# Issuing first-layer and second-layer matmuls alternately in a fused attention and expert-network kernel

## The chip, the cores and the metric

The kernel runs on one core of one Trainium2 chip. It is a single launch that computes everything. The metric is device time in microseconds; three runs of the kernel before gave 687.64, 683.81 and 687.77 us, median 687.64.

## What is computed

The reference has three parts, chained. Retention-like attention over 2 batches, 8 heads, 576 positions, head size 64 gives x, 1152 tokens by 512 features. Then four experts and one more network, each of two layers, run over all tokens:

```python
scores = scale * np.matmul(q, k.transpose(0, 1, 3, 2))
out    = np.matmul(scores * Dmat[None], v)          # Dmat: causal decay
# x is (1152, 512); four experts, w1 (512, 1024), w2 (1024, 512)
h = np.maximum(x @ w1[e], 0.0)
out += p[:, e:e + 1] * (h @ w2[e])
# then one network, w_in (512, 2048), w_out (2048, 512)
h = x @ w_in
sp = np.where(h > 20.0, h, np.log1p(np.exp(np.minimum(h, 20.0))))
g = h * np.tanh(sp)
out = g @ w_out
```

All inputs and outputs are float32.

## The kernel before, in words

**Tiling.** After attention the kernel treats the rest as six experts (EXPERTS): 0 to 3 are the four experts, 4 and 5 the two halves of the last network. Each has 1024 hidden features, cut into 8 units of 128 (UNITS). The 1152 tokens are cut into three chunks of 384 (PH, TC). A *tile* is one unit for one chunk: 24 tiles in an expert (TPE), numbered n = 8 c + t for chunk c and unit t.

**Two layers of a tile.** The first layer (`hidden`) multiplies the weights of the unit with the 512 features of x in four pieces and accumulates 128 hidden features by 384 tokens in one of four banks of PSUM, banks 4 to 7 (`ps_h`), by turns. The second layer (`project`) multiplies the 128 hidden features with the second weights and adds to four output pieces in banks 0 to 3 (`ps_acc`), which collect all eight units of a chunk. Every operand is held as a sum of two parts, `_hi` (rounded) and `_lo` (the rest), so each product is three matmuls of 128x128 by 128x384 (`three`, L265 to L267): hi by hi, hi by lo, lo by hi. A layer of a tile is 4 x 3 = 12 matmuls, all alike in size.

**Between the layers, experts 0 to 3.** VectorE computes relu times the expert's probability out of PSUM (h_act, L531), ScalarE rounds it to h_hi (L416), VectorE subtracts for h_lo (L525). VectorE does this tile by tile (`moe_tile`). After the tile numbered 8 (c+1) + 2, it adds the four accumulators of chunk c to acc_sb (`add_up`, L546, L548).

**Between the layers, experts 4 and 5.** The activation takes more steps: ScalarE m_u (L438), VectorE m_a and m_w (L596, L598), ScalarE m_r twice (L443, L445), GpSimd m_t (L686), VectorE m_c, m_n, h_act (L605, L611, L614), then h_hi and h_lo. The engines are two tiles ahead in a software pipeline. VectorE's order for tile n is

```python
mish_c(n, e)
mish_out(n, e)          # m_n, h_act
mish_w(n + 2, e)        # m_a, m_w of a later tile
lo(n, e)                # h_lo
```

and ScalarE's is m_u of n+2, h_hi of n, m_r of n+2. In the first tile of a chunk `add_up` of the chunk before follows `lo`. GpSimd also makes the low part of each weight unit (w_lo, L191), ScalarE the high part (w_hi, L186), eight of each per expert.

**TensorE's order.** TensorE is three tiles ahead with the first layer (AHEAD): in the loop over experts, chunks and units it issues `hidden` of tile n+3 and then `project` of tile n. I call this pair a *block*. `hidden` waits until its PSUM bank was read (s_hf), and for weights (s_wl) and x (s_ph) where these are new; `project` waits for h_lo (s_hl), and in the first tile of a chunk, before each output piece, until its accumulator was read (s_af). At the end of `hidden` s_g1 is raised, for ScalarE or VectorE; at the end of `project` s_g2. Each engine runs its instructions in the order in which they are written.

Of the kernel before, what the change touches and what calls it, by code (L numbers as in the profile page):

```python
# [29 lines left out]
P = 128  # L30
# [13 lines left out]
UNITS = 8  # L44
EXPERTS = MOE_EXPERTS + MLP_F // (UNITS * P)
TC = 384
PH = TOKENS // TC
TPE = PH * UNITS
KT = DM // P
UW = KT * P + DM  # L50
RAW = 4
HR = 4
# [9 lines left out]
def build(nc, qk_in, kv_in, row_decay_in, key_decay_in, mask_in, probs_in, weights_in, probs_dram, out_t):  # L62
    with ExitStack() as ctx:
        def sb(name, shape, dt=F32, stack=ctx):
            return stack.enter_context(nc.sbuf_tensor(name, shape, dt))

        def sem(name):
            return ctx.enter_context(nc.semaphore(name))
# [5 lines left out]
        x_hi = sb("x_hi", [P, KT, TOKENS], F32R)  # L74
        x_lo = sb("x_lo", [P, KT, TOKENS], F32R)
# [28 lines left out]
        h_hi = sb("h_hi", [P, HR, TC], F32R)  # L104
        h_lo = sb("h_lo", [P, HR, TC], F32R)
# [16 lines left out]
        ps_acc = [banks[d][:, 0:TC] for d in range(KT)]  # L122
        ps_h = [banks[4 + i][:, 0:TC] for i in range(HR)]
# [27 lines left out]
        s_g1 = sem("s_g1")  # L151
        s_acc = sem("s_acc")
        s_g2 = sem("s_g2")
        s_hf = sem("s_hf")
        s_hh = sem("s_hh")
        s_hl = sem("s_hl")
        s_af = sem("s_af")
# [12 lines left out]
        def cols(c):  # L170
            return slice(c * TC, (c + 1) * TC)

        def high(u):
            return w_hi0[:, u] if u < RAW else w_hi1[:, u - RAW]

        def low(u):
            return w_lo0[:, u] if u < RAW else w_lo1[:, u - RAW]
# [72 lines left out]
        @block.tensor  # L250
        def _(pe):
            def scores(b, n):

                slot, par = n % SLOTS, n % 2
                pe.wait_ge(s_qd, 2 * CHUNKS * b + 2 * (n + 1))
                for y in range(2):
                    for i in range(HALF):
                        hp = HALF * y + i
                        mm = pe.matmul(ps_s[par][y][:, i], qk[:, slot, 1, hp, :], q_diag[:, par, hp],  # L259
                                       start=True, stop=True)  # L260
                    mm.then_inc(s_sc, 1)

            def three(out, w, x, first, last):

                pe.matmul(out, w[0], x[0], start=first, stop=False)  # L265
                pe.matmul(out, w[0], x[1], start=False, stop=False)  # L266
                return pe.matmul(out, w[1], x[0], start=False, stop=last)  # L267

            def unit(u, at):

                return high(u)[:, at:at + P], low(u)[:, at:at + P]

            def hidden_products(c, t):

                for k in range(KT):
                    mm = three(ps_h[t % HR], unit(t, P * k), (x_hi[:, k, cols(c)], x_lo[:, k, cols(c)]),
                               k == 0, k == KT - 1)
                mm.then_inc(s_g1, 1)


            pe.wait_ge(s_zt, 1)
            for _ in range(WARM):
                pe.matmul(banks[7][:, :], zeros[:, 0:P], zeros[:, :], start=True, stop=True)
            scores(0, 0)
            with pe.Fori(0, BATCH) as b:
                for c in range(CHUNKS):
                    slot, par = c % SLOTS, c % 2
                    pe.wait_ge(s_vd, CHUNKS * b + c + 1)
                    if c > 0:

                        pe.wait_ge(s_st, 2 * (CHUNKS - 1) * b + 2 * c)
                    if c + 1 < CHUNKS:
                        for hp in range(PAIRS):
                            for x in range(2):
                                head = slice(DH * (2 * hp + x), DH * (2 * hp + x + 1))
                                mm = pe.matmul(ps_state[DH * x:DH * (x + 1), hp, :], kv[:, slot, 0, head],
                                               kv[:, slot, 1, head],
                                               start=(c == 0 and hp == 0), stop=True, skip_group_check=True)
                        mm.then_inc(s_kvp, 1)
                        scores(b, c + 1)  # L300
                    else:
                        with pe.If(b < BATCH - 1):
                            scores(b, c + 1)
                        with pe.If(b == BATCH - 1):


                            pe.wait_ge(s_xl, TC // CH)
                            pe.wait_ge(s_wl, AHEAD)
                            for t in range(AHEAD - 1):
                                hidden_products(0, t)  # L310
                    for y in range(2):
                        pe.wait_ge(s_sm, 2 * CHUNKS * b + 2 * c + y + 1)
                        for hp in range(HALF * y, HALF * (y + 1)):
                            for x in range(2):
                                h = 2 * hp + x
                                mm = pe.matmul(ps_o[par][DH * x:DH * (x + 1), hp, :],  # L316
                                               kv[:, slot, 1, DH * h:DH * (h + 1)],
                                               s_masked[:, par, hp, x, :],
                                               start=(hp == 0), stop=True, skip_group_check=True)
                    if c > 0:  # L320
                        for hp in range(PAIRS):
                            mm = pe.matmul(ps_o[par][:, hp, :], state[:, 1 - par, hp, :], qk[:, slot, 0, hp, :],  # L322
                                           start=False, stop=True, skip_group_check=True)
                    mm.then_inc(s_o, 1)
            pe.drain().then_inc(s_g2, UNITS)
            pe.wait_ge(s_xt, STEPS - 1)
            hidden_products(0, AHEAD - 1)

            def hidden(e, c, t):

                if t == 0:
                    pe.wait_ge(s_ph, PH * e + (c + 1))
                if c == 0:
                    pe.wait_ge(s_wl, UNITS * e + (t + 1))
                pe.wait_ge(s_hf, TPE * e + (UNITS * c + t + 1))
                hidden_products(c, t)

            def project(e, c, t):

                pe.wait_ge(s_hl, TPE * e + (UNITS * c + t + 1))  # L340
                for d in range(KT):
                    if t == 0:
                        pe.wait_ge(s_af, PH * KT * e + (KT * c + d + 1))
                    mm = three(ps_acc[d], unit(t, KT * P + P * d), (h_hi[:, t % HR, :], h_lo[:, t % HR, :]),
                               t == 0, t == UNITS - 1)
                    if t == UNITS - 1 and d < KT - 1:
                        mm.then_inc(s_acc, 1)
                mm.then_inc(s_g2, 1)

            with pe.Fori(0, EXPERTS) as e:  # L350
                for c in range(PH):
                    for t in range(UNITS):
                        n = UNITS * c + t + AHEAD

                        if n < TPE - 1:
                            hidden(e, n // UNITS, n % UNITS)
                        if n == TPE - 2:
                            hidden(e, PH - 1, UNITS - 1)
                        if n >= TPE:
                            with pe.If(e < EXPERTS - 1):  # L360
                                hidden(e + 1, 0, n - TPE)
                        project(e, c, t)


        @block.scalar
# [387 lines left out]
```

## Time and profile before

| | |
|---|---|
| three runs, median | 687.64 us (683.81 to 687.77) |
| profiled execution: span, first to last instruction | 682.0 us (no other time is given for it) |
| attention, loading, first tiles | until about 66 us |
| experts 0 to 3 | about 66 to 467 us |
| experts 4 and 5 | about 467 to 682 us |
| TensorE busy | 657.8 us, 96% |
| VectorE busy | 362.5 us, 53% |
| granted clock of TensorE, mean | 0.997 |

The profile names matmuls by line and operands: `x_hi,w_hi`, `x_lo,w_hi`, `x_hi,w_lo` are first layer, `h_hi,w_hi`, `h_lo,w_hi`, `h_hi,w_lo` second layer; the bank's number is left out. A matmul's length is modelled (0.33 to 0.34 us), and the next one starts before its end, so the distance from start to start, the pitch, is what counts. "Idle before, releaser" in square brackets is how long the engine stood and whose instruction ended it. PEld is the weight load that goes with each matmul.

### The profile page before, as it was taken

What the parts mean: (1) busy time and instruction counts of PE and PEld (TensorE: products, weight loads), DVE (VectorE), ACT (ScalarE), POOL (GpSimd) and SP (SyncE); (2) the same over time, 40 slices, a digit from 0 to 9 for tenths busy, and PEclk for the clock granted to TensorE, in tenths of its full rate; (3) what the DMA queues carried; (4) which work ended last, traced back from release to release, by engine and by line L of the source; (5) the groups of instructions that cost most, each with busy time, mean ns of one, the idle gap of its engine ahead of it and who ended that gap; (6) DMA issues with size and microseconds to landing.
All of it is one profiled execution on the core that took longest, in us unless ns stands there. A gap on an engine that the chain in (4) does not pass through costs nothing.

```text
span 682.0 us, 10838 instructions
## 1 busy us (share of the span) xinstructions
PE 657.8 (96%) x3993; PEld 643.8 (94%) x3993; DVE 362.5 (53%) x618; ACT 225.8 (33%) x405; POOL 187.2 (27%) x113
## 2 busy tenths in 40 slices
PE   8979999999999999999999999999899998799998
PEld 5868999999999999999999999999899997699997
DVE  5534532325232334232344242547997789988786
ACT  4554211133111133111133121235555454444442
POOL 2255400046000056000055000153423256532222
PEclk9989999999999999999999999999999999999999
DMA  9994300023000023000024000031100002001011
GB/s 276 293 281 167 123 1 1 1 93 124 31 0 0 0 92 134 20 0 0 0 93 153 0 0 0 0 122 63 62 0 0 0 31 92 0 0 46 0 46 46
DMA packets 13967, 40.78 MB, mean 60 GB/s; under 512 B 2304, under 2 KB 4608, under 8 KB 13952
## 3 DMA queue, kind: packets, MB, share of 16 engines
q1 hardware_dynamic: 12848, 38.22, 17.5%
q10 hardware_dynamic: 1104, 2.38, 1.1%
q8 instruction: 7, 0.11, 0.1%
q14 instruction: 8, 0.07, 0.0%
HBM read 38.22 MB, written 2.38 MB: 60 GB/s over the span
## 4 chain that ended last, share of the span: by engine, by line
PE 84%; DVE 7%; DMA 4%; ACT 2%; issue 2%; SPq 1%; DVEq 0%; ACTq 0%
PE bank L265 27%; PE bank L267 27%; PE bank L266 27%; DMA qk<-in_qk 4%; DVE m_a L596 3%; PE bank L259 1%; PE bank L322 1%; DVE m_c L605 1%; PE bank L316 1%; DVE m_w L598 1%; ACT m_u L438 1%; ACT w_hi L186 1%; DVE acc_sb L548 1%; ACT m_r L443 1%; DVE h_lo L525 1%
## 5 line engine op out<-in xcount | busy, mean ns | idle before, releaser
L265 PE MATMUL bank<-h_hi,w_hi 128*128 128x384 f32 x576 | 195.4, 339 | 12.9 <-DVE h_lo L525 11.3
L191 POOL TENSOR_TENSOR w_lo<-w_raw,w_hi 128x1024 fp32r<-128x1024 f32 x48 | 117.9, 2461 | 323.0 <-ACT w_hi L186 322.8
L266 PE MATMUL bank<-h_lo,w_hi 128*128 128x384 f32 x576 | 194.0, 337 | 0.0
L267 PE MATMUL bank<-h_hi,w_lo 128*128 128x384 f32 x576 | 194.0, 337 | 0.0
L267 PE MATMUL bank<-x_hi,w_lo 128*128 128x384 f32 x576 | 194.0, 337 | 0.0
L265 PE MATMUL bank<-x_hi,w_hi 128*128 128x384 f32 x576 | 193.7, 336 | 0.1
L266 PE MATMUL bank<-x_lo,w_hi 128*128 128x384 f32 x576 | 193.5, 336 | 0.0
L416 ACT ACTIVATE h_hi<-h_act 128x384 fp32r<-128x384 f32 x144 | 75.2, 522 | 290.2 <-DVE h_act L531 269.0
L531 DVE SCALAR_TENSOR_TENSOR h_act<-bank,pb 128x384 f32<-128x384 f32 x96 | 53.5, 557 | 178.8 <-PE bank L267 178.2
L525 DVE TENSOR_TENSOR h_lo<-h_act,h_hi 128x384 fp32r<-128x384 f32 x144 | 97.4, 676 | 67.2 <-ACT h_hi L416 67.2
L265 PEld LDWEIGHTS bank<-h_hi,w_hi 128*128 128x128 f32 x576 | 108.0, 187 | 16.9 <-DVE h_lo L525 13.8
L265 PEld LDWEIGHTS bank<-x_hi,w_hi 128*128 128x128 f32 x576 | 108.1, 188 | 0.3 <-issue 0.3
L266 PEld LDWEIGHTS bank<-x_lo,w_hi 128*128 128x128 f32 x576 | 108.2, 188 | 0.0
L266 PEld LDWEIGHTS bank<-h_lo,w_hi 128*128 128x128 f32 x576 | 108.1, 188 | 0.0
L267 PEld LDWEIGHTS bank<-x_hi,w_lo 128*128 128x128 f32 x576 | 108.1, 188 | 0.0
L267 PEld LDWEIGHTS bank<-h_hi,w_lo 128*128 128x128 f32 x576 | 108.0, 188 | 0.0
L686 POOL TENSOR_TENSOR m_t<-m_w,m_r 128x384 f32<-128x384 f32 x48 | 56.2, 1171 | 130.1 <-ACT m_r L445 130.1
L186 ACT ACTIVATE w_hi<-w_raw 128x1024 fp32r<-128x1024 f32 x48 | 50.7, 1056 | 34.3 <-PE bank L267 34.2
L596 DVE TENSOR_SCALAR m_a<-m_u 128x384 f32<-128x384 f32 x48 | 37.2, 775 | 29.8 <-ACT m_u L438 29.8
L443 ACT ACTIVATE m_r<-m_w 128x384 f32<-128x384 f32 x48 | 25.2, 526 | 46.6 <-DVE m_w L598 46.6
L438 ACT ACTIVATE m_u<-bank 128x384 f32<-128x384 f32 x48 | 23.3, 485 | 43.6 <-PE bank L267 43.6
L605 DVE SCALAR_TENSOR_TENSOR m_c<-m_r,m_t 128x384 f32<-128x384 f32 x48 | 30.7, 640 | 1.1 <-POOL m_t L686 0.3
(37 smaller groups left out, 321.3 us busy)
## 6 DMA issues: line engine op xcount, KB each, us to landing
w_raw<-in_weights SPq DMA_DIRECT2D x48, 512.0 KB, 3.3
qk<-in_qk SPq DMA_DIRECT2D x12, 384.0 KB, 13.3
kv<-in_kv SPq DMA_DIRECT2D x12, 384.0 KB, 14.6
pb<-probs_by_expert ACTq DMA_DIRECT2D x4, 576.0 KB, 8.9
out_t<-acc_sb SPq DMA_DIRECT2D x2, 768.0 KB, 3.6
row_decay<-in_row_decay SPq DMA_DIRECT2D x6, 192.0 KB, 7.6
out_t<-acc_sb SPq DMA_DIRECT2D x4, 192.0 KB, 1.9
mask<-in_mask SPq DMA_DIRECT2D x1, 36.0 KB, 3.7
```

Source lines behind the costliest of these rows:

```text
L186: act.activation(high(u), w_raw[:, u % RAW, :], ACT.Copy).then_inc(s_wh, 1)
L191: pool.tensor_tensor(low(u), w_raw[:, u % RAW, :], high(u).bitcast(F32), ALU.subtract).then_inc(s_wl, 1)
L265: pe.matmul(out, w[0], x[0], start=first, stop=False)
L266: pe.matmul(out, w[0], x[1], start=False, stop=False)
L267: return pe.matmul(out, w[1], x[0], start=False, stop=last)
L416: act.activation(h_hi[:, n % HR, :], h_act[:, n % 2, :], ACT.Copy).then_inc(s_hh, 1)
L443: act.activation(m_r[:, n % 2, :], m_w[:, n % 2, :], ACT.Ln, bias=2.0).then_inc(s_ln, 1)
L525: dve.tensor_tensor(h_lo[:, n % HR, :], h_act[:, n % 2, :], h_hi[:, n % HR, :].bitcast(F32), ALU.subtract).then_inc(s_hl, 1)
L531: dve.scalar_tensor_tensor(h_act[:, n % 2, :], ps_h[n % HR], 0.0, pb[:, bass.ds(e * TOKENS + (n // UNITS) * TC, TC)], ALU.max, ALU.mult).t ...
L596: dve.tensor_scalar(m_a[:, :], m_u[:, n % 2, :], MISH_CAP, 2.0, ALU.min, ALU.add).then_inc(s_ma, 1)
L605: dve.scalar_tensor_tensor(m_c[:, :], m_r[:, n % 2, :], 2.0, m_t[:, n % 2, :], ALU.mult, ALU.add).then_inc(s_mc, 1)
L686: pool.tensor_tensor(m_t[:, n % 2, :], m_w[:, n % 2, :], m_r[:, n % 2, :], ALU.mult)\
```

## The change

`three` becomes `product`, which issues one of the three matmuls. A new function `both` takes the place of the pair in a block: it does all the waits of both first, then issues first-layer and second-layer matmuls one by one in turns, 24 in all, and raises s_g1 and s_g2 from the last two. Where only one of the two is there, it is issued alone: the first layer of tile 23, the second layer of tile 20, and tiles 21 to 23 of expert 5. The other engines' programs are untouched.

```diff
+            def product(j, out, w, x, first, last):
+                return pe.matmul(out, w[j // 2], x[j % 2], start=first and j == 0, stop=last and j == 2)
...
+            def project_product(e, c, t, d, j):
+                if t == 0 and j == 0:
+                    pe.wait_ge(s_af, PH * KT * e + (KT * c + d + 1))
+                mm = product(j, ps_acc[d], unit(t, KT * P + P * d), (h_hi[:, t % HR, :], h_lo[:, t % HR, :]),
+                             t == 0, t == UNITS - 1)
...
+            def both(e, c, t, he, hc, ht):
+                hidden_ready(he, hc, ht)
+                pe.wait_ge(s_hl, TPE * e + (UNITS * c + t + 1))
+                for i in range(KT):
+                    for j in range(3):
+                        hm = hidden_product(hc, ht, i, j)
+                        pm = project_product(e, c, t, i, j)
+                hm.then_inc(s_g1, 1)
+                pm.then_inc(s_g2, 1)
...
                         if n < TPE - 1:
-                            hidden(e, n // UNITS, n % UNITS)
-                        if n == TPE - 2:
-                            hidden(e, PH - 1, UNITS - 1)
-                        if n >= TPE:
+                            both(e, c, t, e, n // UNITS, n % UNITS)
+                            if n == TPE - 2:
+                                hidden_ready(e, PH - 1, UNITS - 1)
+                                hidden_products(PH - 1, UNITS - 1)
+                        elif n == TPE - 1:
+                            project(e, c, t)
+                        else:
                             with pe.If(e < EXPERTS - 1):
-                                hidden(e + 1, 0, n - TPE)
-                        project(e, c, t)
+                                both(e, c, t, e + 1, 0, n - TPE)
+                            with pe.If(e == EXPERTS - 1):
+                                project(e, c, t)
```

**TensorE, inside a block of chunk 0**, tile 6 (with the first layer of tile 9): before, the end of the first layer and the start of the second. Semaphores in brackets are waited for; `w_hi0`, `w_hi1` are the two halves of the weight store.

```order
L267 MATMUL bank5<-x_hi,w_lo0 128x384
L265 MATMUL bank5<-x_hi,w_hi0 128x384
L266 MATMUL bank5<-x_lo,w_hi0 128x384
L267 MATMUL bank5<-x_hi,w_lo0 128x384
L265 MATMUL bank0<-h_hi,w_hi1 128x384 [waits s_hl]
L266 MATMUL bank0<-h_lo,w_hi1 128x384
L267 MATMUL bank0<-h_hi,w_lo1 128x384
```

The same block now, from its start:

```order
L265 MATMUL bank5<-x_hi,w_hi0 128x384 [waits s_hl,s_hf]
L265 MATMUL bank0<-h_hi,w_hi1 128x384
L265 MATMUL bank5<-x_lo,w_hi0 128x384
L265 MATMUL bank0<-h_lo,w_hi1 128x384
L265 MATMUL bank5<-x_hi,w_lo0 128x384
L265 MATMUL bank0<-h_hi,w_lo1 128x384
L265 MATMUL bank5<-x_hi,w_hi0 128x384
```

The wait for s_hl stood in the middle of the block and now stands before its first matmul, and the two kinds alternate.

**TensorE, the first block of chunk 1** (tile 8, with the first layer of tile 11): before, from the last first-layer matmuls on.

```order
L265 MATMUL bank7<-x_hi,w_hi0 128x384
L266 MATMUL bank7<-x_lo,w_hi0 128x384
L267 MATMUL bank7<-x_hi,w_lo0 128x384
L343 REGISTER_ALU [waits s_hl]
L265 MATMUL bank0<-h_hi,w_hi0 128x384 [waits s_af]
L266 MATMUL bank0<-h_lo,w_hi0 128x384
L267 MATMUL bank0<-h_hi,w_lo0 128x384
```

Now, from the start of the block:

```order
L265 MATMUL bank7<-x_hi,w_hi0 128x384 [waits s_hl,s_hf]
L343 REGISTER_ALU
L265 MATMUL bank0<-h_hi,w_hi0 128x384 [waits s_af]
L265 MATMUL bank7<-x_lo,w_hi0 128x384
L265 MATMUL bank0<-h_lo,w_hi0 128x384
L265 MATMUL bank7<-x_hi,w_lo0 128x384
L265 MATMUL bank0<-h_hi,w_lo0 128x384
```

The wait for the first accumulator (s_af) came after 12 matmuls of the block, and now comes after one.

## Rows read from the trace of the kernel before

**Rows 1.** the page: busy time by engine; chain of waits by engine.

```profile
PE 657.8 (96%) x3993; PEld 643.8 (94%) x3993; DVE 362.5 (53%) x618; ACT 225.8 (33%) x405; POOL 187.2 (27%) x113
...
PE 84%; DVE 7%; DMA 4%; ACT 2%; issue 2%; SPq 1%; DVEq 0%; ACTq 0%
```

**Rows 2.** stretches: length, busy us (count) by engine, granted clock, DMA share, GB/s.

```profile
166.00:267.00 101.00, 101.00 (x579) 101.00 (x579) 36.00 (x62) 20.99 (x32) 19.58 (x8) 1.00 0.12 42
...
467.00:682.00 215.00, 199.89 (x1127) 195.82 (x1125) 179.32 (x313) 102.55 (x201) 80.39 (x57) 1.00 0.08 28
```

**Rows 3.** whom TensorE waited for, 466:682: total, times, longest (us).

```profile
PE bank L265 <- DVE h_lo L525: 10.5, 9, 2.2
PE bank L265 <- DVE acc_sb L546: 1.6, 1, 1.6
```

**Rows 4.** timeline of TensorE, 300 to 312 us: start, length, instruction.

```profile
302.81 0.33 PE L265 MATMUL bank<-h_hi,w_hi 128*128 128x384 f32 x1
...
304.88 0.34 PE L265 MATMUL bank<-x_hi,w_hi 128*128 128x384 f32 x1
...
306.97 0.33 PE L265 MATMUL bank<-h_hi,w_hi 128*128 128x384 f32 x1
...
309.08 0.34 PE L265 MATMUL bank<-x_hi,w_hi 128*128 128x384 f32 x1
```

**Rows 5.** timeline of TensorE, 20 to 60 us: eight 192-column matmuls, twice.

```profile
27.01 1.47 PE L259 MATMUL bank<-q_diag,qk 128*96 128x192 f32 x8
...
36.41 2.87 PE L259 MATMUL bank<-q_diag,qk 128*96 128x192 f32 x8 [2.28 <-ACT q_diag L375]
```

**Rows 6.** timeline of VectorE around a change of chunk, 298 to 304 us.

```profile
298.79 0.56 DVE L531 SCALAR_TENSOR_TENSOR h_act<-bank,pb 128x384 f32<-128x384 f32 x1 [2.51 <-PE bank L267]
...
300.42 1.95 DVE L548 TENSOR_TENSOR acc_sb<-bank,acc_sb 128x384 f32<-128x384 f32 x4
```

**Rows 7.** timeline of one tile, last two experts: start, length, instruction.

```profile
607.07 0.34 PE L267 MATMUL bank<-x_hi,w_lo 128*128 128x384 f32 x1
...
607.44 0.49 ACT L438 ACTIVATE m_u<-bank 128x384 f32<-128x384 f32 x1 [1.61 <-PE bank L267]
...
607.96 0.36 DVE L596 TENSOR_SCALAR m_a<-m_u 128x384 f32<-128x384 f32 x1 [1.14 <-ACT m_u L438]
...
608.83 0.55 DVE L525 TENSOR_TENSOR h_lo<-h_act,h_hi 128x384 fp32r<-128x384 f32 x1
...
610.48 0.56 DVE L614 SCALAR_TENSOR_TENSOR h_act<-bank,m_n 128x384 f32<-128x384 f32 x1
...
611.45 0.34 PE L265 MATMUL bank<-h_hi,w_hi 128*128 128x384 f32 x1
```

**Rows 8.** timeline, 597 to 599.2 us, TensorE starting again after a wait.

```profile
597.25 0.34 PE L267 MATMUL bank<-x_hi,w_lo 128*128 128x384 f32 x1
...
598.12 0.55 DVE L525 TENSOR_TENSOR h_lo<-h_act,h_hi 128x384 fp32r<-128x384 f32 x1
...
598.73 0.44 PE L265 MATMUL bank<-h_hi,w_hi 128*128 128x384 f32 x1 [1.14 <-DVE h_lo L525]
...
599.01 0.34 PE L266 MATMUL bank<-h_lo,w_hi 128*128 128x384 f32 x1
```

**Rows 9.** timeline, 594 to 600 us: GpSimd beside VectorE.

```profile
594.98 2.42 POOL L191 TENSOR_TENSOR w_lo<-w_raw,w_hi 128x1024 fp32r<-128x1024 f32 x1
...
595.07 2.54 DVE L596 TENSOR_SCALAR m_a<-m_u 128x384 f32<-128x384 f32 x1 [0.34 <-ACT m_u L438]
```

**Rows 10.** timeline of TensorE, start of the steady loop, 60 to 76 us.

```profile
64.58 0.33 PE L265 MATMUL bank<-x_hi,w_hi 128*128 128x384 f32 x1
...
67.56 0.44 PE L265 MATMUL bank<-h_hi,w_hi 128*128 128x384 f32 x1 [0.73 <-DVE h_lo L525]
```

**Rows 11.** stretches between 33.5 and 43 us: length, busy us, granted clock.

```profile
36.40:39.80 3.40, 3.38 (x16) 2.67 (x18) 1.58 (x3) 2.21 (x4) 2.70 (x2) 0.50 1.01 258
```

**Rows 12.** busy time by stretch, 574 to 587 us, two whole waits in it.

```profile
574.00:587.00 13.00, 9.28 (x51) 8.32 (x49) 12.30 (x18) 5.68 (x10) 7.01 (x4) 1.00 0.12 40
```

More of the change, by code:

```diff
@@ L261, in scores, with hidden_product @@
                     mm.then_inc(s_sc, 1)
[L263 to L267, printed above, removed]
+            def product(j, out, w, x, first, last):
+                return pe.matmul(out, w[j // 2], x[j % 2], start=first and j == 0, stop=last and j == 2)
             def unit(u, at):
                 return high(u)[:, at:at + P], low(u)[:, at:at + P]
+            def hidden_product(c, t, k, j):
+                return product(j, ps_h[t % HR], unit(t, P * k), (x_hi[:, k, cols(c)], x_lo[:, k, cols(c)]),
+                               k == 0, k == KT - 1)
             def hidden_products(c, t):
                 for k in range(KT):
-                    mm = three(ps_h[t % HR], unit(t, P * k), (x_hi[:, k, cols(c)], x_lo[:, k, cols(c)]),
-                               k == 0, k == KT - 1)
+                    for j in range(3):
+                        mm = hidden_product(c, t, k, j)
                 mm.then_inc(s_g1, 1)
@@ L327, in _, with hidden_ready @@
             hidden_products(0, AHEAD - 1)
-            def hidden(e, c, t):
+            def hidden_ready(e, c, t):
                 if t == 0:
@@ L335, in hidden @@
                 pe.wait_ge(s_hf, TPE * e + (UNITS * c + t + 1))
-                hidden_products(c, t)
+            def project_product(e, c, t, d, j):
[3 more added lines that the diff above has]
+                             t == 0, t == UNITS - 1)
+                if t == UNITS - 1 and d < KT - 1 and j == 2:
+                    mm.then_inc(s_acc, 1)
+                return mm
             def project(e, c, t):
@@ L341, in project @@
                 for d in range(KT):
[L342 to L347, printed above, removed]
-                mm.then_inc(s_g2, 1)
+                    for j in range(3):
+                        mm = project_product(e, c, t, d, j)
+                mm.then_inc(s_g2, 1)
+            def both(e, c, t, he, hc, ht):
+                hidden_ready(he, hc, ht)
+                pe.wait_ge(s_hl, TPE * e + (UNITS * c + t + 1))
+                for i in range(KT):
+                    for j in range(3):
+                        hm = hidden_product(hc, ht, i, j)
+                        pm = project_product(e, c, t, i, j)
+                hm.then_inc(s_g1, 1)
+                pm.then_inc(s_g2, 1)
             with pe.Fori(0, EXPERTS) as e:
```

## The prediction, written before the result was known

> **What bounds the kernel now.** I read the page's busy times and its chain of waits first. TensorE is busy for 657.8 of 682.0 us, and 84% of the chain that ended last is TensorE [rows 1]. So the time is the number of matmuls by their pitch, plus whatever TensorE waits. The stretches then split the program. While experts 0 to 3 run, TensorE is busy all the time: 579 matmuls in 101.00 us is 174.4 ns each [rows 2]. From 467 us on (experts 4 and 5, the second network) it is busy for 199.89 of 215.00 us [rows 2], and the table of waits names h_lo nine times and acc_sb once, 12.1 us together [rows 3]. So there are two questions: does the pitch of 174.4 ns change, and which waits does the new order make?
>
> **The pitch.** The change wants neighbouring matmuls to write different banks. The old order holds both cases already. In a first-layer group of 12 matmuls every neighbour writes the same bank; in a second-layer group of 12 the bank changes every third matmul, and once more on leaving it. The groups start at 302.81, 304.88, 306.97 and 309.08 [rows 4]: 2.07 us and 2.11 us for two second-layer groups, 2.09 us for the first-layer group between them. Four changes of bank save nothing that can be read; the scatter allows 5 ns each, either way. So I price the alternation at 0. The alternating stretches hold 135 blocks of 24 matmuls (23 tiles in each of experts 0 to 4, 20 in expert 5), 3,240 in all. On the bad side 5 ns each are +16 us. For the good side the nearest row is another long f32 matmul: eight of 192 columns, 0.33 us each like these, take 1.47 us, a pitch of (1.47 - 0.33) / 7 = 163 ns [rows 5]. Were that the floor here too, 11 ns by 3,240 are -36 us. (Those eight write one bank four in a row, which is again no sign that a shared bank costs anything.)
>
> The Trainium skill (TensorE: Matmul & The Clock Gate, Back-to-back issue gap) states N/2.4 + 2.5 ns for a warm engine, 162.5 ns here. The measured 174.4 is 12 ns more; if same-bank neighbours were the reason, the sum would be 39 us lower. The second-layer groups, which change banks and are no shorter, speak against that.
>
> **The waits.** The old block of tile n is: first-layer matmuls of tile n+3, a wait for h_lo of n, second-layer matmuls of n. The new one waits for h_lo of n before its first matmul, and the first layer of n+3 ends with the block. So h_lo is wanted 12 matmuls (2.09 us) earlier, and the first-layer result comes 12 matmuls later: 4.2 us less room between them. In experts 0 to 3 this is covered: VectorE starts h_act at 298.79 and is past h_lo at 300.42, 1.63 us later [rows 6], and two blocks, 8.4 us, are left.
>
> **Experts 4 and 5 lose the cover.** VectorE and ScalarE work there in a software pipeline: VectorE does m_a and m_w of tile n+2 *before* h_lo of n, and these need m_u of n+2, which needs the first layer of n+2. The new order issues that in the block of n-1, to its very end, and block n begins with the wait for h_lo of n. So the whole chain lies bare between two blocks. The rows give its length: the last first-layer matmul starts at 607.07, m_u at 607.44, m_a at 607.96, h_lo (behind m_w) at 608.83, ending at 609.38 [rows 7]. In the old order the matmul that needs it starts at 611.45 [rows 7], 2.07 us later: that margin was the group which now has no place there. After h_lo TensorE takes 0.06 us to start (598.67 to 598.73), and the next matmul follows 0.28 us on instead of 0.17 [rows 8], 0.10 us more. The next block would have started two pitches after 607.07, at 607.42. It will start at 609.44: 2.02 + 0.10 = **2.12 us lost in each block**.
>
> How many: tiles 0 to 19 of both experts, and 22 and 23 of expert 4 (expert 5 has no tile n+2 left there): 42. For tiles 20 and 21 the first layer of tile 23 and the second layer of 20 are issued apart. 42 x 2.12 = **+89.0 us**. The rest of VectorE's work (m_c, m_n, h_act) follows h_lo; h_act starts 1.65 us after it (608.83 to 610.48) [rows 7], so it fits under the 4.19 us of matmuls, and the cycle is 4.19 + 2.12 = 6.31 us.
>
> The waits that are there now are replaced: 12.1 us of idle time in 10 waits [rows 3], each with 0.16 us by which the shown length of a matmul (0.34) passes its pitch, and 0.10 us of restart: **-14.8 us**. They came from GpSimd's w_lo, beside which m_a takes 2.54 us [rows 9] instead of 0.36 [rows 7]. In the new cycle w_lo starts about 3.7 us after the first layer ends (behind m_w, two m_r and m_t) and takes 2.4 us, so it is over before the next m_a at 6.7 us.
>
> Smaller terms there, all estimates from the same rows: the first tile of each chunk also waits for the first addition out of the accumulators, 0.3 us, six times: +1.8. In the first tile of each expert the four additions (1.95 us [rows 6]) push m_c into w_lo: 2 x 0.5 = +1.0. Tiles 20 to 23: VectorE's three instructions for tile 21 stand between h_lo of 20 and m_a of 23, so h_lo of 21 is about 1 us late in either expert, and the last two tiles of expert 5 are 0.8 us late: +2.8. Sum **+5.6 us**.
>
> **A wait at each change of chunk.** In experts 0 to 3 VectorE empties the accumulators only after h_act and h_lo of a tile whose first layer used to end 4.2 us before the new chunk's second layer. Now it ends with the block before it. An engine follows the matmul's end by 0.03 us (607.41 to 607.44) [rows 7]; the first addition starts 1.63 us after h_act (298.79 to 300.42) and takes 0.49, a quarter of 1.95 [rows 6]; with 0.06 us to TensorE and the matmul's own 0.34 that is 2.55 us after the last first-layer matmul's start, against three pitches, 0.52. Lost: 2.03 + 0.10 = 2.13 us. There are 11 such changes before expert 4 (its own is in the 42): **+23.4 us**. The later additions come 0.49 us apart, before the 1.05 us of their six matmuls.
>
> **The start.** Now the first layer of tile 3 starts at 64.58, under the wait for tile 0's h_lo, which ends at 67.56 [rows 10]. It will start with that wait: 12 matmuls, **+2.1 us**.
>
> Sum: 682.0 + 89.0 - 14.8 + 5.6 + 23.4 + 2.1 = **787.3 us** for an execution like the profiled one. The median of the three times shown, 687.64, is 5.6 us above that span. Forecast: **793 us**, 15% slower.
>
> **The rivals.**
> 1. *The collisions with w_lo stay.* If the 10 stretched instructions still fall on the bare chain, each adds what it costs now, 14.8 us together: 808 us. For it: VectorE is busy for 179 of the 215 us [rows 2]. Against it: the phases above. Chance 0.12.
> 2. *The chain is only partly bare*, because blocks or order are not as I read them: half of the 89.0 and 23.4 us, so 737 us. Against it: h_lo stands right behind m_w in [rows 7]. Chance 0.05.
> 3. *The clock falls.* It does once, to half, in a stretch of 3.4 us [rows 11] right after an idle 2.28 us, and eight matmuls then take 2.87 instead of 1.47 us [rows 5], so such a stretch loses some 1.6 us. One in each of the 42 blocks: +67, 860 us. Against it: in the new cycle TensorE works 4.4 of 6.3 us, 70%; between 574 and 587 us it was busy for 9.28 of 13.00, 71%, with two whole waits of about 2 us, and the granted clock stayed 1.00 [rows 12]. Chance 0.05. The Trainium skill (TensorE: Matmul & The Clock Gate, A second HAM failure mode: psum-queue depth-cycling) tells of a kernel that cycles through banks and loses its clock again and again in the small gaps between matmul groups; by it the time would lie at this rival's. The stretch from 574 us does not agree.
> 4. *The other side: matmuls of two banks overlap more.* Each is shown for 0.34 us at a pitch of 0.17 [rows 4], so two are under way at once. If accumulation into one bank held the second back, alternating would cut the pitch in all 135 blocks. It decides from (787.3 - 682.0) / 3,240 = 33 ns a matmul on; at 35 ns the time is 680 us, no slower than before. Against it: [rows 4] once more, and a pitch of 140 ns is under any of these long f32 matmuls, 163 [rows 5]. Chance 0.02. The smaller form, 11 ns less and the same waits, gives 757 us: chance 0.05.
> 5. *The order does not change on TensorE.* The instruction orders shown above exclude it.
>
> **How the numbers follow.** The forecast has the remaining 0.71. Its 2.12 us may be off by 0.2 in each of 53 waits, 11 us either way, and the offset of span and median may be 2 instead of 5.6: 778 to 804. Rival 1 takes the top to 812; below, the smaller pitch and a part of rival 2 reach to 768. **Range 768 to 812**. With 1% as what a measurement of this kernel can tell from no change, only rival 4's first form is not slower: slower 0.98, same 0.01, faster 0.01.
>
> **What the new profile would show.** In experts 4 and 5 some 42 waits of TensorE for h_lo, each about 1.9 us of idle time (2.02 less 0.16, plus a little where acc_sb ends it), a cycle of 6.3 us, m_a near 0.36 us nearly everywhere; 11 waits for acc_sb before; a pitch of 174 ns inside a block; clock 1.00. If the pitch inside a block is 163 ns or less, the bank mattered; if the waits are there but under 1.5 us, I have misread the pipeline; if the chunk changes show none, VectorE's order there is not what I took it to be.

## The result

| | before | changed |
|---|---|---|
| runs, median | 686.04 us (4 runs, 683.81 to 687.77) | 834.51 us (4 runs, 829.01 to 835.65) |
| profiled execution, span | 682.0 us | 832.0 us |
| granted clock, mean | 0.997 | 0.946 |

The changed kernel takes 1.214 times as long (95% interval 1.209 to 1.220). The forecast was 793 us with a range up to 812: the direction was right, the size was not. 148 us came instead of 107.

### The profile page after: what moved, and what is told of

Its sections match the earlier page's. It is cut to its first block, busy times and chain, and to the rows that moved or that the text cites. A ratio compares the mean times of both kernels' runs of the same rounds, so it can differ in the third digit from the quotient of the medians.

```text
span 832.0 us, 10973 instructions
## 1 busy us (share of the span) xinstructions
PE 707.5 (85%) x3993; PEld 677.9 (81%) x3993; DVE 338.6 (41%) x618; ACT 223.6 (27%) x405; POOL 186.0 (22%) x113
## 4 chain that ended last, share of the span: by engine, by line
PE 52%; issue 30%; POOL 9%; DMA 4%; DVE 2%; ACT 1%; SPq 1%; DVEq 0%; POOLq 0%; ACTq 0%
PE bank L265 50%; POOL m_t L709 6%; DMA qk<-in_qk 4%; POOL w_lo L191 3%; PE bank L259 1%; DVE h_act L554 1%; DVE acc_sb L571 1%; ACT h_hi L439 1%; PE bank L325 1%; PE bank L319 0%; DVE h_lo L548 0%; SPq L211 0%; SPq L208 0%; SPq L207 0%; DVE acc_sb L569 0%
## 5 line engine op out<-in xcount | busy, mean ns | idle before, releaser
L265 PE MATMUL bank<-x_hi,w_hi 128*128 128x384 f32 x576 | 204.2, 355 | 88.9 <-DVE h_lo L548 88.8
L265 PE MATMUL bank<-h_hi,w_hi 128*128 128x384 f32 x576 | 204.0, 354 | 22.7 <-DVE acc_sb L571 15.4
L265 PE MATMUL bank<-h_lo,w_hi 128*128 128x384 f32 x576 | 202.0, 351 | 0.0
L265 PE MATMUL bank<-x_lo,w_hi 128*128 128x384 f32 x576 | 201.2, 349 | 0.0
L265 PE MATMUL bank<-x_hi,w_lo 128*128 128x384 f32 x576 | 200.2, 348 | 0.0
L265 PE MATMUL bank<-h_hi,w_lo 128*128 128x384 f32 x576 | 200.2, 348 | 0.0
L265 PEld LDWEIGHTS bank<-h_lo,w_hi 128*128 128x128 f32 x576 | 114.2, 198 | 0.0
L265 PEld LDWEIGHTS bank<-x_hi,w_lo 128*128 128x128 f32 x576 | 114.1, 198 | 0.0
L548 DVE TENSOR_TENSOR h_lo<-h_act,h_hi 128x384 fp32r<-128x384 f32 x144 | 87.6, 609 | 57.3 <-ACT h_hi L439 57.3
L619 DVE TENSOR_SCALAR m_a<-m_u 128x384 f32<-128x384 f32 x48 | 19.6, 408 | 149.6 <-ACT m_u L461 149.6
```

What stands on the lines that cost most here:

```text
L265: return pe.matmul(out, w[j // 2], x[j % 2], start=first and j == 0, stop=last and j == 2)
L548: dve.tensor_tensor(h_lo[:, n % HR, :], h_act[:, n % 2, :], h_hi[:, n % HR, :].bitcast(F32), ALU.subtract).then_inc(s_hl, 1)
L619: dve.tensor_scalar(m_a[:, :], m_u[:, n % 2, :], MISH_CAP, 2.0, ALU.min, ALU.add).then_inc(s_ma, 1)
```

## The profile after

The page first: TensorE's busy time, the clock in 40 slices of the span (tenths), and the chain that ended last by engine.

```profile
PE 707.5 (85%) x3993; PEld 677.9 (81%) x3993; DVE 338.6 (41%) x618; ACT 223.6 (27%) x405; POOL 186.0 (22%) x113
...
PEclk9979999999999999999999999999999989999999
...
PE 52%; issue 30%; POOL 9%; DMA 4%; DVE 2%; ACT 1%; SPq 1%; DVEq 0%; POOLq 0%; ACTq 0%
```

TensorE still executes 3,993 matmuls. Its busy time rose from 657.8 to 707.5 us [rows 1]. Each wait adds a little to it (0.16 us by which a shown length passes the pitch, and 0.1 us of restart), some 12 us for 57 waits less the ten old ones. The rest of the 50 us means longer matmuls, that is a slower clock. (The share of "issue" in the chain, 30%, is time that this view could not give to anything; the waits have to be read elsewhere.) The table of waits gives the other part.

```profile
PE bank L265 <- DVE acc_sb L571: 15.4, 8, 1.9
PE bank L265 <- DVE acc_sb L569: 5.8, 3, 1.9
PE bank L265 <- DVE h_lo L548: 2.7, 1, 2.7
```

and from 500 us on:

```profile
PE bank L265 <- DVE h_lo L548: 87.6, 45, 3.3
```

In experts 0 to 3 there are the 11 waits for the first addition, 21.2 us, and one at the start. In experts 4 and 5 there are 45 for h_lo, 87.6 us; before it was nine and one, 12.1 us [rows 3]. One of them in the timeline of all engines (start, length, instruction):

```profile
741.04 0.34 PE L265 MATMUL bank<-h_hi,w_lo 128*128 128x384 f32 x1
741.24 0.49 ACT L461 ACTIVATE m_u<-bank 128x384 f32<-128x384 f32 x1 [4.03 <-PE bank L265]
...
741.76 0.36 DVE L619 TENSOR_SCALAR m_a<-m_u 128x384 f32<-128x384 f32 x1 [1.45 <-ACT m_u L461]
...
742.63 0.55 DVE L548 TENSOR_TENSOR h_lo<-h_act,h_hi 128x384 fp32r<-128x384 f32 x1
...
743.33 0.42 PE L265 MATMUL bank<-x_hi,w_hi 128*128 128x384 f32 x1 [1.95 <-DVE h_lo L548]
...
743.59 0.34 PE L265 MATMUL bank<-h_hi,w_hi 128*128 128x384 f32 x1
```

These lines answer to [rows 7] and [rows 8]. The last matmul of the block starts at 741.04. The last one of the first layer, one before it, ends just before 741.24, m_u follows, h_lo ends at 743.18 (742.63 + 0.55), and the next block starts at 743.33. From 741.04 to 743.33 are 2.29 us instead of 0.17, and the restart costs 0.09 more: 2.20 us lost, forecast 2.12. The steps from the matmul to h_lo took what [rows 7] had; the 0.08 us more lie between h_lo's end and the next matmul, 0.15 us here against the 0.06 of [rows 8]. m_a takes 0.36 us; over all 48 tiles its mean fell from 775 to 408 ns. GpSimd's w_lo now runs while VectorE stands idle, and is over before the next m_a:

```profile
528.05 2.42 POOL L191 TENSOR_TENSOR w_lo<-w_raw,w_hi 128x1024 fp32r<-128x1024 f32 x1
...
530.86 0.36 DVE L619 TENSOR_SCALAR m_a<-m_u 128x384 f32<-128x384 f32 x1 [3.24 <-ACT m_u L461]
```

Then the clock. Three stretches of 13 us, nearly the same place:

```profile
740.00:753.00 13.00, 9.10 (x51) 8.52 (x51) 6.25 (x13) 3.90 (x8) 2.43 (x2) 1.00 0.12 44
743.40:756.40 13.00, 9.09 (x50) 8.52 (x51) 6.20 (x13) 4.15 (x9) 2.43 (x2) 1.00 0.00 0
746.00:759.00 13.00, 9.09 (x45) 8.52 (x44) 5.94 (x12) 3.90 (x8) 2.42 (x2) 0.90 0.00 0
```

The clock fell to half at 756.4, so the second stretch is what TensorE did just before, and the third, with a clock of 0.90, has the fall in it. The shares of busy time are the same, 70%, and like that of [rows 12]: before the fall TensorE did what it also did in the first stretch, behind whose waits the clock stayed (in the third the same share stands for fewer matmuls, 45 instead of 51, since they are longer at half clock). Close up after a wait at a change of chunk that ended at 110.98, the timeline of TensorE (start, length):

```profile
111.28 0.52 PE L265 MATMUL bank<-x_lo,w_hi 128*128 128x384 f32 x1
111.60 0.52 PE L265 MATMUL bank<-h_lo,w_hi 128*128 128x384 f32 x1
...
114.16 0.52 PE L265 MATMUL bank<-h_hi,w_lo 128*128 128x384 f32 x1
...
114.91 0.33 PE L265 MATMUL bank<-x_lo,w_hi 128*128 128x384 f32 x1
115.08 0.34 PE L265 MATMUL bank<-h_lo,w_hi 128*128 128x384 f32 x1
```

and the row of the stretches for it, with the granted clock third from the end:

```profile
111.15:114.55 3.40, 3.40 (x12) 3.40 (x13) 1.17 (x3) 0.00 (x0) 0.00 (x0) 0.51 0.00 0
```

From 111.28 to 114.16 the pitch is 320 ns (nine matmuls, 2.88 us), from 114.91 on 170 again. The record of the granted clock in this trace holds 22 such stretches of 3.4 us at half clock inside the loop; each begins between the end of a wait and 1.5 us after it. In the kernel before, the loop has none. One follows the wait at the start, ten follow the 11 changes of chunk, and 11 lie in experts 4 and 5. In 3.4 us at 320 ns there are 10.6 matmuls instead of 19.5: a stretch loses 8.9 x 0.174 = 1.55 us.

The sum over the profiled execution: 682.0, + 42 x 2.20 = 92.4, + 11 x 2.18 = 24.0 (2.25 us from matmul to matmul at the changes of chunk, less 0.17, plus 0.10), - 14.8 + 5.6 + 2.1 as forecast, + 22 x 1.55 = 34.1, + 6.1 since the first h_lo came 6.1 us later in this execution (the attention part lies before the changed loop and also moves from run to run): 831.5 us. Measured 832.0; 0.5 us are left open. The line for the 6.1 us, beside 67.56 in [rows 10]:

```profile
73.62 0.65 PE L265 MATMUL bank<-x_hi,w_hi 128*128 128x384 f32 x1 [2.69 <-DVE h_lo L548]
```

## Experiments

Each is compared with runs of the kernel before on the same chip (median 685.2 us for e1 to e4, 687.2 for e5 to e8, 687.7 for e9 to e11). The clock is that of the profiled execution.

| run | what it is | us | ratio to before, 95% | clock |
|---|---|---|---|---|
| changed kernel | | 834.5 | 1.214 (1.209 to 1.220) | 0.946 |
| e1 | waits as changed, order in groups | 837.4 | 1.222 (1.214 to 1.230) | 0.959 |
| e2 | changed, waits filled with 11 matmuls | 798.2 | 1.165 (1.157 to 1.173) | 0.996 |
| e9 | changed, waits filled with 5 | 800.2 | 1.166 (1.162 to 1.171) | 0.989 |
| e3 | alternating in experts 0 to 3 only | 730.4 | 1.061 (1.052 to 1.070) | 0.967 |
| e4 | alternating in experts 4 and 5 only | 789.0 | 1.149 (1.139 to 1.158) | 0.965 |
| e10 | changed, additions one tile earlier | 794.4 | 1.157 (1.151 to 1.163) | 0.965 |
| e5 | changed, h_lo before m_a | 758.9 | 1.102 (1.096 to 1.108) | 0.951 |
| e6 | both of these | 718.7 | 1.047 (1.043 to 1.052) | 0.983 |
| e8 | both, first layer four tiles ahead | 699.6 | 1.019 (1.014 to 1.024) | 0.985 |
| e7 | both, on the order of before | 690.5 | 1.005 (1.001 to 1.009) | 0.995 |
| e11 | before, w_lo shortened in experts 4, 5 | 673.2 | 0.982 (0.977 to 0.987) | 0.992 |

### Is it the alternation or the waits? (e1)

```diff
                 for i in range(KT):
                     for j in range(3):
-                        hm = hidden_product(hc, ht, i, j)
                         pm = project_product(e, c, t, i, j)
-                hm.then_inc(s_g1, 1)
+                for i in range(KT):
+                    for j in range(3):
+                        hm = hidden_product(hc, ht, i, j)
                 pm.then_inc(s_g2, 1)
+                hm.then_inc(s_g1, 1)
```

> Edit: in each block of both layers the waits stay where the change put them (h_lo before the first matmul), but the matmuls go in two groups: first the 12 of the second layer, then the 12 of the first, so neighbours share a bank as before. Theory 1 (the time is the bare chain between blocks plus the clock stretches that follow the waits; banks do nothing): the first layer still ends with the block, so the same 53 waits of about 2 us stay, some 20 stretches of 3.4 us at half clock too: 820 to 845 us, within 2% of the changed kernel, pitch 174 to 176 ns. Theory 2 (alternating itself costs or gives time, in the pitch or by the order): the time moves off the changed kernel's by more than 15 us, and the pitch with it.

837.4 us (833.1 to 841.9), 3 us above the changed kernel; the runs of the two overlap. Not one pair of neighbours inside the first layer changes its bank here, and the time is the same. What both have in common is where the waits stand. The profiled executions agree more closely than the medians: e1's has 12.6 us more idle time in the waits, three low stretches fewer (19 instead of 22 in the loop, 4.7 us less), and its first h_lo came 7.5 us sooner. From 832.0 us that gives 832.4; its span is 831.3. In this run's timeline the last first-layer matmul starts at 741.15 and the next block at 743.61, 2.46 us: 0.17 more than in the changed kernel, since there the first layer ends one matmul before the block does.

```profile
741.15 0.34 PE L265 MATMUL bank<-x_hi,w_lo 128*128 128x384 f32 x1
743.61 0.41 PE L265 MATMUL bank<-h_hi,w_hi 128*128 128x384 f32 x1 [2.13 <-DVE h_lo L550]
```

### Is it the clock? (e2, e9)

```diff
             def both(e, c, t, he, hc, ht, fill=True):
                 hidden_ready(he, hc, ht)
+                for _ in range(11 if fill else 0):
+                    pe.matmul(ps_h[ht % HR], zeros[:, 0:P], zeros[:, 0:TC], start=True, stop=True)
                 pe.wait_ge(s_hl, TPE * e + (UNITS * c + t + 1))
```

`fill` is true in every block of experts 4 and 5, and in experts 0 to 3 (in a loop of their own) in the first block of each chunk. e9 has 5 in the place of 11.

> Edit: the changed kernel, with 11 matmuls of zeros (128x384, into the free bank of the coming first layer) issued before the wait for h_lo in every block of experts 4 and 5, and in the first block of each chunk in experts 0 to 3; about 1.8 us each time, under the wait. Theory 1 (the clock falls because TensorE stands still in the waits): the 23 low stretches after the start of the loop go, each giving back about 1.6 us, so about 37 us less than the changed kernel: 790 to 803 us, mean clock above 0.98. Rival (the low stretches come from something else, such as the amount of work, or the extra over the forecast is not the clock): clock near 0.95 and 830 us or more.

798.2 us: 36.3 less than the changed kernel, by doing 605 matmuls more (bf16 zeros, 11 in each of 55 places). No low stretch is left in the loop. (The 23 of the expectation counted one at the very end of the kernel, behind the loop; it is 22.)

```profile
PE 770.8 (97%) x4598; PEld 696.5 (88%) x4598; DVE 338.2 (43%) x618; ACT 223.6 (28%) x405; POOL 185.7 (23%) x113
...
PEclk9989999999999999999999999999999999999999
```

The chains between blocks are as long as before (from h_lo to h_lo 6.34 us against 6.41, medians of the last two experts); only the clock is different. That leaves 798.2 - 685.2 = 113 us for the waits, where the forecast's terms had 105.

> Edit: as the run with 11 matmuls of zeros before the waits, but with 5, so that TensorE still stands idle for about 1.1 us in each of the 53 places instead of 2. Theory (the low clock stretches follow the long idle times): shortening them to 1.1 us is enough, 795 to 806 us and mean clock above 0.98. Rival (any idle time at these places brings the same number of low stretches, filled or not): about 20 of them, 830 us.

800.2 us. TensorE stands idle in 57 places here too, 1.1 us each in the mean:

```profile
PE bank L265 <- DVE h_lo L567: 50.4, 46, 2.3
PE bank L265 <- DVE acc_sb L590: 8.7, 8, 1.1
PE bank L265 <- DVE acc_sb L588: 3.3, 3, 1.1
```

Only two low stretches are left in the loop, and they follow its longest idle times, one at the start and one near the change from expert 4 to 5 (2.3 us, the longest in the rows). None of the 55 others, 0.6 to 1.5 us long, is followed by one. So in this kernel idle times of 1.9 us and more were followed by them in part of the cases, and those of up to 1.5 us in none.

### Which part of the program? (e3, e4)

```diff
-            with pe.Fori(0, EXPERTS) as e:
+            with pe.Fori(0, MOE_EXPERTS) as e:
...
+            with pe.Fori(M0, EXPERTS) as e:
```

The first loop issues its blocks by `both` in e3 and by `hidden`, then `project` in e4; the second loop the other way round.

> Edit: matmuls alternate only in experts 0 to 3; experts 4 and 5 have the order of before, in a loop of their own. Theory 1: 11 waits of 2.13 us, 2.1 us at the start, and about 10 low stretches of 1.6 us: 686 + 23.4 + 2.1 + 16 = 728 us (720 to 738). Theory 2 (the loss is proportional to alternating matmuls): 92 of 135 blocks would carry 68% of the 148 us, 787 us.

> Edit: matmuls alternate only in experts 4 and 5; experts 0 to 3 have the order of before. Theory 1: 42 waits of 2.12 us, less the 14.8 us of old waits, plus 5.6 us, plus about 13 low stretches of 1.6 us: 686 + 89.0 - 14.8 + 5.6 + 21 = 787 us (775 to 797). Theory 2 (loss proportional to alternating matmuls): 43 of 135 blocks, 733 us.

730.4 and 789.0 us. The losses, 45 and 104 us, add up to 149, the whole 148. 68% of the alternating matmuls carry 30% of the loss. That excludes a loss in proportion to the alternating matmuls and fits the count of waits. The low stretches are 11 in e3 (12 new waits) and 13 in e4 (45 waits).

### Taking the waits away (e10, e5, e6)

e10, in VectorE's program for experts 0 to 3 (its two other loops over AHEAD tiles, and ScalarE's second rounding of x, are shifted by one in the same way):

```diff
-                    for n in range(UNITS * c + AHEAD, UNITS * (c + 1) + AHEAD):
+                    for n in range(UNITS * c + AHEAD - 1, UNITS * (c + 1) + AHEAD - 1):
```

> Edit: the changed kernel, with only the accumulators' additions one tile earlier in experts 0 to 3. Theory 1 (the 11 waits at the changes of chunk are this order): they go with their low clock stretches, 834.5 - 23.4 - 16 = 795 us (787 to 803); the low stretches in experts 4 and 5 stay. Rival (the low stretches of experts 0 to 3 are not from these waits): 811 us.

794.4 us, 40 less, with no wait for acc_sb left. The waits at the changes of chunk, and the low stretches behind them, come from VectorE's order in the changed kernel.

e5, in VectorE's program for experts 4 and 5 (the additions of a chunk's first tile stand where the "..." is), and in ScalarE's:

```diff
                         mish_out(n, e)
-                        if n + 2 < TPE:
-                            mish_w(n + 2, e)
+                        lo(n, e)
...
-                        lo(n, e)
+                        if n + 2 < TPE:
+                            mish_w(n + 2, e)
...
-                            mish_exp(n + 2, e)
                             hi(n, e)
+                            mish_exp(n + 2, e)
```

> Edit: the changed kernel, in experts 4 and 5 VectorE makes h_lo of tile n before m_a and m_w of n+2 (and the accumulators' additions right behind h_lo), ScalarE h_hi of n before m_u of n+2. So block n no longer waits for anything that needs the first layer of tile n+2. Theory 1 (the 42 waits are this order and nothing else): they go, and with them the clock stretches there; what stays is the loss of experts 0 to 3, 730 us, less the old 14.8 us of waits, plus a residue where w_lo meets the chain: VectorE's work from m_a of n+1 to h_lo of n takes some 3.8 us of the 4.2 us block, so the 11 tiles with w_lo may each wait about 1 us: 720 to 750 us. Rival (the alternating order leaves VectorE and ScalarE too little time in whatever order): over 770 us.

758.9 us: above the range that I gave, but 76 us below the changed kernel, so most of the 42 waits were the order of m_a and h_lo. The expectation priced the residue too low: 15 waits for h_lo stay, 1.9 us in the mean, the start's among them, and three of the low stretches, which began in its longest waits (2.95 to 3.5 us), lasted 6.8 us, twice as long as those of the changed kernel.

```profile
PE bank L265 <- DVE h_lo L547: 28.0, 15, 3.5
```

e6 has both edits.

> Edit: as the run before, and in experts 0 to 3 VectorE adds up the accumulators one tile earlier, before it turns to the tile whose first layer has just ended (ScalarE's second rounding of x one tile earlier with it). Theory 1: the 11 waits at the changes of chunk go too, and nearly all low clock stretches: 686 + 2.1 - 14.8 + 0 to 25 for the residue at w_lo = 675 to 700 us. If alternating banks saved 11 ns a matmul it would be 36 us less than that; if it cost something by itself, more than the same fix on the order of before plus 25.

718.7 us, again above. The residue at w_lo was taken for 0 to 25 us; it is 15 waits of 26 us in sum, the start's among them, with five low stretches after the start's. The next run shows where part of it comes from; its waits of 2.1 to 3.5 us were not taken apart.

### Without alternation, and four tiles ahead (e7, e8)

e7 is the edits of e6 on the kernel before.

> Edit: both of VectorE's and ScalarE's new orders, on the kernel before, with its two groups of 12 matmuls in each block. Theory 1: the ten old waits (14.8 us) in experts 4 and 5 go, since h_lo no longer stands behind the m_a that w_lo stretches: 686 - 14.8 = 671 us (668 to 676). Rival (the old waits have another cause): 683 us or more. This is the base for what alternating does when nothing waits.

690.5 us: **the expectation failed**. The waits in experts 4 and 5 are still there, 14.3 us where they were 12.1, and one low stretch follows. In the timeline of GpSimd and VectorE they have only moved to another instruction.

```profile
560.30 2.40 POOL L191 TENSOR_TENSOR w_lo<-w_raw,w_hi 128x1024 fp32r<-128x1024 f32 x1
...
560.64 2.47 DVE L524 TENSOR_TENSOR h_lo<-h_act,h_hi 128x384 fp32r<-128x384 f32 x1 [0.86 <-ACT h_hi L416]
563.04 0.35 DVE L595 TENSOR_SCALAR m_a<-m_u 128x384 f32<-128x384 f32 x1
563.42 0.56 DVE L597 SCALAR_TENSOR_TENSOR m_w<-m_u,m_a 128x384 f32<-128x384 f32 x1
563.90 0.55 DVE L604 SCALAR_TENSOR_TENSOR m_c<-m_r,m_t 128x384 f32<-128x384 f32 x1
564.48 0.56 DVE L610 SCALAR_TENSOR_TENSOR m_n<-m_c,m_t 128x384 f32<-128x384 f32 x1
565.07 0.56 DVE L613 SCALAR_TENSOR_TENSOR h_act<-bank,m_n 128x384 f32<-128x384 f32 x1
566.49 2.47 DVE L524 TENSOR_TENSOR h_lo<-h_act,h_hi 128x384 fp32r<-128x384 f32 x1 [0.86 <-ACT h_hi L416]
```

Now it is h_lo that takes 2.47 us while w_lo runs, where it was m_a [rows 9]. From h_lo to h_lo are 5.85 us, and a block of matmuls takes 4.19. VectorE is busy for 5.0 us of them and waits 0.86 for h_hi. In the tiles with a w_lo it has too much to do, in either order.

e8 is e6 with the first layer one tile further ahead on TensorE (the other engines keep three):

```diff
-AHEAD = 3
+AHEAD = 4
...
-                            for t in range(AHEAD - 1):
+                            for t in range(AHEAD - 2):
...
+            hidden_products(0, AHEAD - 2)
+            pe.wait_ge(s_xt, STEPS)
             hidden_products(0, AHEAD - 1)
```

> Edit: alternating order with both fixes, and the first layer four tiles ahead instead of three. So each first-layer result has the 4.2 us again that the alternating order took. Theory 1: no waits but the start's; the time is the pitch alone, so within 1% of the pair kernel with the same fixes, 668 to 680 us. Theory 2 (alternating banks shortens the pitch): 11 ns by 3,240 matmuls less, 636 us; (it lengthens the pitch): 5 ns more, 690 us.

699.6 us, 9 above e7 and 20 above the end of what theory 1 allowed: a residue stays here too, 17 waits for h_lo of 19.6 us in sum and three low stretches (e7: 15.0 us of waits in all, and one). But the pitch can now be read in experts 0 to 3, where almost nothing waits (three waits of 0.2 us, one of them in the stretch below). The same stretch in e7 (groups) and e8 (alternating):

```profile
166.00:267.00 101.00, 101.00 (x579) 101.00 (x578) 37.99 (x61) 20.88 (x32) 19.61 (x8) 1.00 0.13 42
```

```profile
166.00:267.00 101.00, 100.80 (x578) 100.48 (x577) 46.18 (x61) 20.31 (x32) 19.36 (x9) 1.00 0.13 42
```

579 matmuls in 101.00 us of work, and 578 in 100.80: 174.4 ns both, the number of [rows 2]. Alternating the banks neither gave nor cost a nanosecond here.

### The old waits (e11)

```diff
+        def short_lo(pool, e, u):
+            pool.wait_ge(s_wh, UNITS * e + (u + 1))
+            pool.tensor_tensor(low(u)[:, 0:16], w_raw[:, u % RAW, 0:16], high(u)[:, 0:16].bitcast(F32),
+                               ALU.subtract).then_inc(s_wl, 1)
...
-                            unit_lo(pool, e, UNITS - LAG + t)
+                            short_lo(pool, e, UNITS - LAG + t)
...
-                                unit_lo(pool, e + 1, t - LAG)
+                                short_lo(pool, e + 1, t - LAG)
```

> Leaves out: 15/16 of each w_lo that is made while experts 4 and 5 run (16 of 1024 columns are made, 128x16), on the kernel before. Theory (the ten old waits come from VectorE being held while GpSimd makes w_lo, whatever VectorE's order): they all go, 686 - 14.8 = 671 us, m_a 0.36 us in all tiles. Rival (they come from VectorE's own work or from ScalarE's w_hi): 683 us or more.

The kernel leaves out 15/16 of these w_lo. 673.2 us, 14.5 less than before. One wait of 0.8 us is left after 66 us, at the start:

```profile
PE bank L271 <- DVE h_lo L531: 0.8, 1, 0.8
```

So the size of that term, 14.8 us, is confirmed. It is no kernel to use, since w_lo is needed. No version that computes everything beat the kernel before: e7, the nearest, takes 0.5% longer (0.1 to 0.9).

## Why the prediction was right and wrong

**Right: the pitch.** Priced at 0 from [rows 4]; e1 and the pair e7, e8 show 0 within a nanosecond. Both forms of rival 4 are excluded.

**Right: the waits.** 42 of 2.12 us forecast, 2.20 measured; 11 of 2.13 forecast, 2.18 measured. Together 116.4 against 112.4 us. The cycle is 6.39 us (743.33 to the next block's start at 749.72), forecast 6.31. The mechanism (h_lo of n behind m_a of n+2, behind the end of the block; the first addition behind the newest tile) is shown by e5 and e10, which change VectorE's and ScalarE's order alone.

**Right: the old waits go.** -14.8 us (the working, 12.1 and 10 x 0.26, gives 14.7); e11 gained 14.5. The changed kernel's m_a is short in nearly all tiles because its cycle of 6.4 us leaves VectorE room, and w_lo falls into its idle time, as the prediction had it. That e7 did not gain the same on the order of before shows that the reason was the amount of work, not the order of two instructions, as I had thought after the result.

**Wrong: rival 3, the clock.** This is the step that failed: the forecast's sum has nothing for the clock, and it measured 34.1 us. I gave the rival 0.05 and ruled it out by one stretch, [rows 12]: 71% busy, "two whole waits of about 2 us", clock 1.00. That reading was wrong as well. The stretch holds one wait of 0.49 us, one of 1.61 and the first 1.6 us of the next, which ended after it:

```profile
574.87 0.45 PE L265 MATMUL bank<-h_hi,w_hi 128*128 128x384 f32 x1 [0.49 <-DVE h_lo L525]
...
580.94 0.44 PE L265 MATMUL bank<-h_hi,w_hi 128*128 128x384 f32 x1 [1.61 <-DVE acc_sb L546]
...
587.53 0.44 PE L265 MATMUL bank<-h_hi,w_hi 128*128 128x384 f32 x1 [2.15 <-DVE h_lo L525]
```

In its loop the kernel before has a single wait as long as the new ones, that of 2.15 us. So the evidence against the rival was one wait. The changed kernel has stretches with the same busy share at 1.00 and at 0.90, and of its 55 waits of 1.9 us and more 22 are followed by a low stretch. The evidence that I put aside was [rows 11]: one idle time of 2.28 us in the attention part with the clock at half right after it. The price per stretch was well sized (1.6 us forecast, 1.55 by the timeline, 36.3 / 22 = 1.65 by e2); its number was the mistake, in both directions: not 0, not 42, but 22. A middle case, half of the waits followed, would have been 793 + 26 x 1.6 = 835 us, but only hindsight gives that share. The rule of the Trainium skill that I had set against [rows 12] (TensorE: Matmul & The Clock Gate, A second HAM failure mode: psum-queue depth-cycling), small gaps between groups and a clock that goes up and down, agrees with the changed kernel, where the clock fell 22 times. What makes the gaps here is not which banks the matmuls write: e1, whose first-layer neighbours share a bank, has them too, and e5 and e10 take them away by VectorE's and ScalarE's order.

**Wrong: the range.** It followed from the same step: 812 held the rival of the w_lo collisions, which did not stay on the bare chain, and none of the clock's. Of the 44.7 us between the sum (787.3) and the measured span (832.0), 34.1 are the clock, 4.0 the waits, 6.1 the later end of the attention part.

**Offset.** The 5.6 us between span and median were no fixed cost: the changed kernel's profiled execution took 833.9 us with a span of 832.0, 1.9 us more. The other 3.7 us were the spread between executions.

## What to carry to other kernels

Before interleaving two streams of work on one engine, write down for each what it waits for and who waits for its end: merged, both begin with the later wait and both end with the block, and a pipeline that had room on each side can lose it all. A trace that has the two cases side by side, here same-bank and other-bank neighbours, answers the question of the gain without a run. When an edit adds idle time to TensorE of about 2 us at a time, count on the clock for a share of it, and do not clear it by one or two waits that happened to go well; if the waits can't be avoided, matmuls of zeros into a free bank are a cheap filler.

## What the runs showed of the hardware

- In the changed kernel an idle time of TensorE of 1.9 to 3.3 us was followed by 3.4 us at half clock in 22 of 55 cases; the busy share of the stretch before it did not tell which, and the longest was not among them. Over the loops of all 13 traces, 104 of 244 idle times of 1.8 to 3.5 us were followed by a fall of the clock, or had one in them, and none of 126 between 0.4 and 1.8 us. With the waits filled (e2) there was none. Matmuls of zeros kept the clock up here.
- The share differs by place: ten of 11 equal waits in experts 0 to 3, 37 us apart, but 11 of 45 (two of them under 0.9 us) in experts 4 and 5; in e1, 11 of 11 and 7 of 45. Why was not tried.
- VectorE's h_lo, which reads two tiles in SBUF, took 2.47 us beside GpSimd's w_lo and 0.55 us alone. The Trainium skill (SBUF — State Buffer, SBUF: two separate sides) says that such an instruction and a GpSimd one that reads SBUF lock a shared pair of ports for their whole length; e7's rows agree: w_lo runs from 560.30 to 562.70, and h_lo, started beside it, ends 0.41 us after it. m_a, with one input, was held too (2.54 against 0.36 us). Where the two met tile after tile, VectorE's 5.85 us a tile set the pace, not TensorE's 4.19.
